# Four small reorderings and 68 products that nobody reads, in a fused attention, MLP and expert kernel

## What is computed

```python
# attention: 4 batches, 8 heads of 64, 576 keys
scores = q @ k.T / 8
mask   = scores >= (32nd largest of the row)
attn   = softmax(where(mask, scores, -1e9))
x      = attn @ v
# MLP
h = x @ w_in                      # 512 -> 2048
g = max(h, 0) + log1p(exp(-abs(h)))
x = g @ w_out                     # 2048 -> 512
# experts: 8, top 1
logits = x @ w_gate
out[t] = p[best] * (max(x[t] @ w1[best], 0) @ w2[best])
```

## Time and profile before

| | |
|---|---|
| median of 3 runs | 1065.46 us (1063.24 to 1065.86) |
| the profiled execution | 1067.26 us; span of its instructions 1065.0 us |
| TensorE (PE) busy | 994.3 us, 93% |
| VectorE (DVE) | 817.9 us, 77% |
| ScalarE (ACT) | 726.6 us, 68% |
| GpSimd (POOL) | 712.0 us, 67% |
| chain that ended last | PE 83%, ACT 6%, DVE 3%, issue 3% |
| mean granted TensorE clock | 0.965 |
| gathers `xs<-x_rows` | x19, median 3.4 us from issue to landing |

### The profile page before, as it was taken

How to read it: one execution, slowest core, us unless ns; L and a number is a source line. 1 busy time by engine, 2 the same in 40 slices (tenths; PEclk the granted TensorE clock), 3 DMA queues, 4 the chain that set the end, 5 groups by cost and what they waited for, 6 DMA issues and landing times.

```text
span 1065.0 us, 21464 instructions
## 1 busy us (share of the span) xinstructions
PE 994.3 (93%) x6878; PEld 809.2 (76%) x6879; DVE 817.9 (77%) x1744; ACT 726.6 (68%) x1390; POOL 712.0 (67%) x831
## 2 busy tenths in 40 slices
PE   3556799999999999999999999999999999999996
PEld 1344678788788888888878888888887788888875
DVE  7899999999999999999989999994254622222261
ACT  2878788888998998998888998998555111111140
POOL 2688988889899899899888899899352312111101
PEclk9855899999999999999999999999999999999999
DMA  9722235353334543432444332433481421111100
GB/s 309 244 99 99 99 117 171 104 170 114 122 111 151 159 149 124 139 120 86 164 169 135 132 110 100 134 120 113 150 326 70 166 86 48 49 39 39 39 20 20
DMA packets 43390, 130.98 MB, mean 123 GB/s; under 512 B 4320, under 2 KB 18656, under 8 KB 33056
## 3 DMA queue, kind: packets, MB, share of 16 engines
q1 hardware_dynamic: 40256, 120.09, 32.5%
q0 software_dynamic: 3040, 9.70, 2.8%
HBM read 111.95 MB, written 18.09 MB: 122 GB/s over the span
## 4 chain that ended last, share of the span: by engine, by line
PE 83%; ACT 6%; DVE 3%; issue 3%; POOL 2%; DMA 1%; SPq 1%; ACTq 0%; DVEq 0%; POOLq 0%
PE psum L604 8%; PE psum L565 7%; PE psum L634 7%; PE psum L579 7%; PE psum L727 6%; PE psum L729 6%; PE psum L728 6%; PE psum L653 6%; PE psum L636 6%; PE psum L635 6%; PE psum L655 6%; PE psum L654 6%; PE psum L759 2%; PE psum L676 1%; DMA wo_raw<-in_moe_w_out 1%
## 5 line engine op out<-in xcount | busy, mean ns | idle before, releaser
L1140 DVE MAX8 top<-work 128x8 f32<-128x576 f32 x432 | 304.7, 748 | 0.0
L1146 DVE MATCH_REPLACE8 work<-top,work 128x576 f32<-128x576 f32 x288 | 212.2, 746 | 0.0
L634 PE MATMUL psum<-x_parts,wi_hi 128*128 128x256 f32 x576 | 171.1, 297 | 0.0
L635 PE MATMUL psum<-x_parts,wi_hi 128*128 128x256 f32 x576 | 163.0, 283 | 0.0
L636 PE MATMUL psum<-x_parts,wi_lo 128*128 128x256 f32 x576 | 162.9, 283 | 0.0
L1515 POOL TENSOR_SCALAR pr<-sc,top 128x576 f32<-128x576 f32 x64 | 142.5, 2226 | 6.4
L604 PE MATMUL psum<-prT,vtok 128*64 128x128 f32 (+3 forms) x1600 | 117.1, 287 | 11.2 <-ACT prT L905 11.2
L604 PEld LDWEIGHTS psum<-prT,vtok 128*64 128x64 f32 (+1 forms) x1600 | 85.6, 144 | 50.6 <-issue 41.1
L1620 POOL DMA_INDIRECT out<-ys,dst_now x19 | 19.2, 1012 | 156.5 <-DVE ys L1342 154.5
L565 PE MATMUL psum<-kT,qT 64*128 64x512 f32 (+3 forms) x640 | 111.2, 474 | 13.5 <-ACT sc L877 8.9
L1511 POOL TENSOR_TENSOR pr<-sc,pr 128x576 f32<-128x576 f32 x80 | 114.3, 1433 | 11.3 <-ACT pr L885 11.3
(11 more groups left out here) (206 smaller groups left out, 2259.5 us busy)
## 6 DMA issues: line engine op xcount, KB each, us to landing
wo_ring<-wo_parts SPq DMA_DIRECT2D x72, 1024.0 KB, 4.9
wo_parts<-wo_ring SPq DMA_DIRECT2D x8, 1024.0 KB, 3.8
kT<-in_k SPq DMA_DIRECT2D x16, 288.0 KB, 3.7
qT<-in_q SPq DMA_DIRECT2D x16, 288.0 KB, 3.9
vtok<-in_v SPq DMA_DIRECT2D x16, 256.0 KB, 2.9
wo_raw<-in_moe_w_out SPq DMA_DIRECT2D x1, 4096.0 KB, 14.0
wi_raw<-in_moe_w_in SPq DMA_DIRECT2D x4, 1024.0 KB, 14.5
x_rows<-x2tok SPq DMA_DIRECT2D x16, 256.0 KB, 2.5
```

The lines of the kernel that those rows point to most:

```text
L634: nc.tensor.matmul(ps[:, part, :], wi_hi[:, u, kk, f], hi, start=first, stop=False)
L635: nc.tensor.matmul(ps[:, part, :], wi_hi[:, u, kk, f], lo, start=False, stop=False)
L1140: nc.vector.max(top[:, at, 8 * r:8 * r + 8], sc[:, at, :] if r == 0 else work[:, t, :]).then_inc(topk_step, 1)
L1146: nc.vector.match_replace(work[:, t, :], top[:, at, 8 * r - 8:8 * r], sc[:, at, :] if r == 1 else work[:, t, :], TAKEN).then_inc(topk_step, 1)
```

## The change

It does four things.
- ScalarE's step before 10: probs_out(i-2) goes behind exponentials(i-1).
- TensorE's steps 6 to 9: `fill` issues 5 products behind the scores, 4 behind the transposes, and 8 behind times_v. Each is an identity of 128 x 128 by itself in fp32, into bank 7 of PSUM, which nobody reads before `down` and starts anew there.
- VectorE's reciprocals from block 9 on go one round up: ahead of the maxima of round 1.
- Behind the loop: count_late goes from its place ahead of turn_xs(1) into e_up(1), behind its first three matmuls; slots_late goes in e_down(0) from ahead of product 3 to ahead of product 5, behind turn_h(1); ScalarE does gate_exps(1) after ReLU and xs_out(1); VectorE does relu(0) before it waits for the last logits, and xs_low(1) before gates.

```diff
--- before.py
+++ after.py
@@ -612,6 +612,13 @@
             def k_last(g):
                 return KD - 1 if PIECES[2 * g + 1][0] == "full" else KD // 2
 
+
+
+            def fill(i, many):
+                if MLP_AT - 4 <= i < MLP_AT:
+                    for _ in range(many):
+                        nc.tensor.matmul(psum[:, 7, 0:P], ident[:], ident[:], start=True, stop=True)
+
             def up(g, u, amid=()):
                 n = UNITS * g + u
                 steps_x = PAIRS * 2 * (g + 1)
@@ -792,10 +799,12 @@
                     amid[0, k_last(up_at(i)[0])] = lambda: scores(i + AHEAD)
                 elif is_block(i + AHEAD):
                     scores(i + AHEAD)
+                    fill(i, 5)
                 if up_at(i):
                     up(*up_at(i), amid)
                 if late:
                     turn_probs(i - 2)
+                    fill(i, 4)
                 if i in TURNS:
                     turn_tokens(*TURNS[i], 0)
                 if i in LOGITS:
@@ -805,6 +814,7 @@
                         down(*down_at(i), part)
                 if late:
                     times_v(i - 2)
+                    fill(i, 8)
 
             def last_down(u):
                 for part in range(2):
@@ -841,11 +851,10 @@
                                  (1, 2): lambda: turn_tokens(LASTG, NT - 1, 4),
                                  (1, 3): lambda: logits(NT - 2, 3)}, halves=True, parts=(1,))
             logits(NT - 1, 7)
-            count_late()
             turn_xs(1, 1)
             turn_h(0)
-            e_up(1, rank_first)
-            e_down(0, 0, rank_first, {KE // 2 - 1: slots_late, KE // 2: lambda: turn_h(1)}, halves=True)
+            e_up(1, rank_first, {(0, 1): count_late})
+            e_down(0, 0, rank_first, {KE // 2: lambda: turn_h(1), KE // 2 + 1: slots_late}, halves=True)
             e_down(1, 1, rank_first, {KE - 2: lambda: turn_xs(2, 2)})
             pe.wait_ge(tiles_ready, 1)
             e_up(2)
@@ -1033,13 +1042,13 @@
                         for t in cuts(i - 1):
                             cut_off(i - 1, t)
                     scores_out(i + AHEAD)
-                    if late:
-                        probs_out(i - 2)
                     if wo_unit(i) is not None:
                         split_wo(wo_unit(i))
                     if now:
                         exponentials(i - 1, 0)
                         exponentials(i - 1, 1)
+                    if late:
+                        probs_out(i - 2)
                     if wi_unit(i) is not None:
                         split_wi(wi_unit(i))
                     continue
@@ -1106,9 +1115,9 @@
             logits_out(NT - 2, 3)
             logits_out(NT - 1, 7)
 
-            gate_exps(1)
             e_relu_out(0)
             xs_out(1)
+            gate_exps(1)
             e_h_out(0, 0)
             e_relu_out(1)
             e_h_out(1, 1)
@@ -1165,7 +1174,7 @@
                     for t in range(2):
                         if r:
                             strike(n, t, r)
-                    if r == 2 and n > MLP_AT:
+                    if r == 1 and n > MLP_AT:
                         reciprocals(n - 2)
                     for t in range(2):
                         maxima(n, t, r)
@@ -1367,11 +1376,11 @@
             first_w2(0)
             first_w2(1)
 
+            relu(0)
             dve.wait_ge(logits_copied, NT)
             choose(LAST, 1)
-            relu(0)
+            xs_low(1)
             gates(LAST, 1)
-            xs_low(1)
             dve.wait_ge(counts_ready, 2)
             then(nc.vector.tensor_copy(new_count[:].rearrange("p t e -> p (t e)"),
                                        psum[:, 7, 2 * E:4 * E]))
```

## The result

| | before | changed |
|---|---|---|
| median of 6 runs each | 1065.66 us (1063.24 to 1068.03) | 1058.43 us (1056.75 to 1059.99) |
| profiled execution, span | 1067.26, 1065.0 | 1057.05, 1054.8 |
| ratio of the runs | 1 | 0.9931, 95% interval 0.9916 to 0.9946 |

The changed kernel is 7.2 us faster by the medians, 10.2 by the two profiled executions. The forecast was 9.6 (1055.9). I take the mechanism first, by the profiles, and then these 3 us.

What follows compares the result with a forecast made beforehand. VectorE, waiting in a ring with ScalarE, was taken to bound the first 130 us, TensorE the rest. Front 8.4 plus tail 1.2 gave 9.6 us less: 1057.7 profiled, 1055.9 median; range 1053.0 to 1060.7.

Steps and rivals of the forecast that it cites:

- The bound and the ring: Steps up to 9: VectorE waits in a 10.93 us ring through ScalarE; exponentials first make it 9.89, VectorE 5.2 us earlier.
- signs of being wrong: ScalarE waiting at masks, fillers ahead of a waited-for scores product, or ScalarE standing for biases in steps 12 to 16.
- The front: Up to times_v of block 9, at 128.4 where it was 136.9: gain 8.4 us, 9.0 if the clock holds.
- its own branch: Likeliest case: TensorE's clock falls shortly after its step 9 stop, from 104.6 to 107.35, and returns with unbroken work.
- The limit by VectorE: Tightest at block 14, slack 3.9 to 4.2 us; any front gain over 9.4 would be cut off.
- The earlier reciprocals: Blocks above 10: block 9's reciprocal 2.77 us earlier; later 7.0 instead of 4.2 us of top-k behind each stop, hidden.
- The tail: Behind the loop: reordering removes TensorE's 1.29 us wait and the halved clock; gain 1.2 us (0 to 2).
- The fillers: 17 unread products in each of steps 6 to 9, 0.23 us each at full clock; worth -0.5 to +0.5, put at 0.
- rival A: Fillers cost more, 0.44 us each, or half clock lasts longer: gain about 6.8, 1058.7 us; chance 0.13.
- The size: Whole kernel: 8.4 + 1.2 = 9.6 us gain; 1057.7 for a profiled execution, median 1.8 under it, 1055.9.

Runs made afterwards that it cites:

- exps_only: Before with only ScalarE's new order in steps before 10, exponentials ahead of copied probabilities: 1060.03 us, ratio 0.9945.
- after_again: The changed kernel, unedited, run again beside before on another chip: 1058.23 us, ratio 0.9937.
- cut9: Changed kernel with FREE = MLP_AT - 1, so block 8 too gets a cut-off on ScalarE for both tiles: 1056.27 us, ratio 0.9915.
- recip_only: Before with only the reciprocals of blocks above 10 moved ahead of the maxima of round 1: 1063.02 us, ratio 0.9967.
- nine_cut9_early: Changed kernel without step 9's last eight products, with FREE = MLP_AT - 1 and block 0's exponentials ahead of w_out's split: 1054.11 us, ratio 0.9895.
- parts of 12.4: The change's four parts (ScalarE's order, reciprocals, unread products, tail), each alone against before: 5.9, 3.5, 1.8 and 1.2 us less, in sum 12.4.
- no_fill: Changed kernel without any of its unread products: 1057.04 us, ratio 0.9924.
- tail_only: Before with only the reordering behind the loop: 1064.93 us, ratio 0.9989.
- no_eight_9: Changed kernel without the last eight unread products, those of step 9 ahead of the first up: 1056.47 us, ratio 0.9922.

## Why the prediction was right or wrong

**The bound and the ring: right.** Reciprocals 9.9 apart, the first wait left, times_v(7) at 107.07 (forecast 107.35), exponentials done 6.6 us after the reciprocal (7.0), and no stop before block 9's transposes. `exps_only` shows the largest part of it alone. One of the signs of being wrong did appear, at little price: ScalarE waits at the masks, 2.1 us at block 8, as foreseen, and 0.4 in each of blocks 10 to 13, which was not.

**The front: right, and in its own branch.** The forecast had the clock fall in step 9: times_v(8) at 118.8, block 9's transposes at 124.6, its times_v at 128.4. `after_again`, where it fell, has 118.85, 124.80 and 128.83. In the first profile it held, and they are at 117.47, 123.42 and 127.45; 9.4 us gained there, 9.0 forecast. (136.9 less 128.4 is 8.5 and not 8.4.)

**The limit by VectorE: right in kind, and the most useful step.** I gave 9.4 as the most that the front could take. The profile has 9.4 with 0.6 us left in block 15, so the limit lay near 10 (`cut9`, which stands at it, has 9.9): VectorE had come 5.5 us forward and not 5.2. `recip_only`, `cut9` and `nine_cut9_early` each ran into the limit visibly. It does not explain why parts of 12.4 make 7.2, for the whole had 0.6 us to spare in both of its profiles. What the runs do show are the eight products (1.8) and the overlap at block 9; no run splits the difference further.

**The earlier reciprocals: the price right, its form wrong.** I wrote that VectorE's stops for POOL's sums would be longer. They are not (14.6 us for 18.2); what shrank is the slack, to 1.5 us at the tightest, where 1.4 was forecast. Not in the sum at all is the stop of 1.44 us at block 9 when the clock had fallen; whether it costs anything by itself no run shows.

**The tail: 1.0 to 1.2 for 1.2**, with turn_h(1)'s wait at 0.89 (1.1) and the third gather still hidden.

**The fillers: the price right, the worth wrong.** 0.23 us a product holds: at full clock eight took 1.81 us to the next start. By the rule of the Trainium skill (TensorE: Matmul & The Clock Gate, section Terms), by which I priced them in rival A, eight would have taken 3.5 us, an estimate; the traces don't agree. But I wrote that all of them together are worth 0. They cost 1.2, by `no_fill`. The term that failed is "Without fillers the first up would start at 109.9 at half and the second would end near 124". `no_fill`'s profile has times_v(7) at 106.76, the first up at 109.13, and a granted clock of 0.50 up to 110.40 and 1.00 from there, within that first up: without fillers the work itself raises it just as soon. So the second up was over before 122.85, when block 9's transposes start.

**The size: 9.6 forecast, 7.2 measured, in the range.** The term that was mis-sized is the step from a profiled execution to the median. The sum was made against the profiled execution of before and came to 1057.7 for a profiled one of the change; that one took 1057.05. Then it took off 1.8 for the median, as before's profile lay 1.8 over its median then (1.6 over that of six runs). The change's profile lay 1.4 under its own, and 1.6 and 1.4 are the 3 us between the two readings. Both have to do with the clock: before's profiled execution had its half clock for longer than another of the same front (block 20 at 243.72 against 242.51 in `tail_only`), and after's is one in which it held (234.30 against 235.63). Against `tail_only`'s front the 8.4 of the forecast would have been 7.2; at block 20 the two executions of the change have 8.2 and 6.9 there. The second term is the fillers' worth, put at 0 where `no_fill` has a cost of 1.2. That 9.6 less these two is just 7.2 is chance: each is read from one or two executions, and the runs of one kernel scatter by up to 5 us. It is chance too that rival A's 1058.7 lies nearer to the result than the forecast: its condition, 0.44 us a product at full clock and steps over 9.9, is in no trace.

## What to carry to other kernels

When an engine's pause is removed, look first for the slack of the next one in the same rows: it tells the most that all such edits can give together, and their gains alone don't add up. Work that only keeps a clock up belongs where the engine would otherwise wait anyway, if anywhere: there it gained at most 1.1 us (`nine_cut9_early`) or nothing that could be told (`no_eight_9` against `no_fill`), and ahead of the first instruction of the long stretch eight products cost 1.8. And a clock that stands at half, or doesn't, in the one profiled execution is a sample: price it from more than one.

## What was not expected of the hardware

The same program's TensorE clock falls or doesn't after stops of about the same length. In the changed kernel it held through a stop of 2.52 us in one execution and fell behind one of 2.28 in the next. In before's tail it fell behind one of only 1.29 us, after work at full clock: 1.00 from 812 to 817.4 us, 0.50 from 820 to 822. Before's front, behind stops of 2.82 and 2.74, had a mean granted clock of 0.56 from 130 to 137 us in one execution and of 0.76 in the other. The two kernels with products whose stop ahead of times_v(7) is only 0.77 us (`cut9`, `nine_cut9_early`), where the clock held in the profile, had the least scatter: their runs lie within 0.42 and 0.25 us, those of the other kernels within 0.56 to 5.2. That is a hint and no more, with 4 and 5 runs against up to 24, and `after_again`'s five, where it fell, within 0.56.
